# First loads padded by the host, decays and output weights first on the SyncE queue, gate columns copied by VectorE

## The chip, the cores and the metric

The kernel runs on one core of a Trainium2 chip. The time is device microseconds for one execution of the whole program, and the median of several executions is quoted. The profiled execution is one further run, with a time of its own.

## The reference

Three stages in float32 follow each other. The first is a linear recurrence over 768 steps for 4 batches and 8 heads of size 48:

```python
cur = einsum('bhd,bhe->bhde', u[None] * kt, vt)
y[:, :, t] = einsum('bhd,bhde->bhe', rt, state + cur)
state = wt[:, :, :, None] * state + einsum('bhd,bhe->bhde', kt, vt)
```

The second takes the 3072 resulting rows of 384 numbers through a dense layer: `a = x @ w1`, `b = x @ w2`, `h = a * b @ w3`, `h @ w_out`. The third is a mixture of 8 experts with a noisy top-2 choice: `logits = x @ w_gate`, `noise_scale = log1p(exp(x @ w_noise))`, and for each token the two largest of `logits + noise_scale * noise` choose the experts, each `relu(x @ w1[e]) @ w2[e]`, added with softmax weights.

## The kernel before, in words

**Attention.** Two heads make a pair (HP = 4 pairs a batch); head h of a pair lies on partitions 64h to 64h+47, since HB = 64 and D = 48. For each pair the kernel loads the decays w, the keys k and the receptance r turned (48 rows of 768 time steps a head) into `wt`, `kt`, `rt`, each with two buffers. The rows 48 to 63 of both heads are never loaded; a clearing at the start writes 1.0 over the whole of all six buffers (VectorE the three first buffers at L618, GpSimd the three second ones at L611), and the first load of a buffer waits for its clearing (`turned_clear`, L145). The time axis is cut into NC = 6 chunks of 128. VectorE scans the decays (`dve_decays`, L257), takes their inverse (L268), forms `kdiv` (L275) and `rdec` (L281), and from the row tiles `kn` and `rn` the diagonal `diag` (L292, L298, L307). ScalarE spreads `diag` over `att` (L320), TensorE makes the scores in two halves (L189), VectorE masks them into `att` (L328). TensorE turns the keys (L198), ScalarE copies them to `kend_t` (L248), TensorE multiplies them with the values (`pe_state`, L210), and states and outputs follow (L234, L240).

**The start-up.** While the first batch's attention runs, the weights are prepared. w3 and w_out are multiplied ahead of time, together with 2E = 16 gate columns. `front` does: six turns of w_out blocks (`wo_turn`, L655, copied by ScalarE to `woT`, L575), the product of w_out with the gate matrices (`wo_gates`, L664, copied at L583), and the turning back of that (`gates_turn`, L671), which ScalarE copies into the columns DM to WA of `wo` (L586, raising `wo_ready`). `build` then has 32 quarters `w3_mm` (L679): eight blocks `w3T` of w3, two buffers, each block in four quarters of two matmuls. The block q + 2 is loaded after the last quarter of block q (L545), in SyncE's program order, so behind other loads.

**Order.** All engines run lists written out at build time. `threaded` puts the main steps between attention slots; every engine walks the same list in the same order and does its own share of each step. At the start the list is: derive 0 (scan), two turns, derive 1, a turn, derive 2, a turn, derive 3 and 4, two turns, derive 5, diag 0, `wo_gates`, diag 1 and 2, four spreads, `gates_turn`; then the scores' first half, the turned keys, the first w3 quarter, the scores' second half, the state product, and so on. So ScalarE's copy of the gate columns comes behind the four spreads of three ACTIVATE each, and the second half of the scores comes behind the first w3 quarter on TensorE.

**Queues.** SyncE issues nearly all transfers, in one order: wt, kt, rt of pair 0, w3T block 0, kn, rn, u, the values, w3T block 1, the same of pair 1 with the first w1 blocks. ScalarE issues w_out (two halves of 768 KB) and the gate matrices on its own queue at the very start.

After the first batch the group loop begins (L793 and L810: the dense layer, with the attention of the next batch between), and then the experts (L1222, L1238).

Of the kernel before, what the change touches and what calls it, by code (L numbers as in the profile page):

```python
# [5 lines left out]
B, H, S, D = 4, 8, 768, 48  # L6
DM = H * D
# [50 lines left out]
def program(nc, w_turned, k_turned, r_turned, k_rows, r_rows, v_rows, u, w1, w2, w3_turned, w_out, gate_rows, noise_rows, ew1, ew2_rows, out):  # L58
# [10 lines left out]
    with top:  # L69
# [49 lines left out]

        xr_loaded = [asem("xr_loaded0")]  # L120
        consts_ready, ident_ready, small_loaded, pad_zero = (sem(x) for x in ("consts_ready", "ident_ready", "small_loaded", "pad_zero"))
        turned_clear = [sem(f"turned_clear{i}") for i in range(2)]
        ones_ready, cleared = sem("ones_ready"), sem("cleared")
        pool_waited = sem("pool_waited")
        loaded = [[sem(f"{x}_loaded{i}") for i in range(2)] for x in "wkr"]
# [15 lines left out]

        def sp_input_load(sp, b, q, n):
            g, i = HP * b + q, q % 2
            if g < 2:
                sp.wait_ge(turned_clear[g], n + 1)  # L145
            else:
                sp.wait_ge((decay_ready, kdiv_ready, rdec_ready)[n], g - 1)
            for h in range(2):
                sp.dma_start((wt, kt, rt)[n][i][h * HB:h * HB + D, :],
                             (w_turned, k_turned, r_turned)[n][bass.ds(b, 1), 2 * q + h, :, :].rearrange("o d t -> (o d) t")  # L150
                             ).then_inc(loaded[n][i], 16)

        def sp_rows_load(sp, b, q):
# [338 lines left out]
        with ExitStack() as ph:  # L492
# [24 lines left out]
            def first_sp(sp):  # L517
                def load_w3(n):
                    need(sp, wa_full, n - 1)
                    sp.dma_start(w3T[n % 2][:, :, :].rearrange("p m j -> p (m j)"), w3_turned[n, :, :]).then_inc(w3_loaded[n % 2], 16)  # L520

                def load_w12(n):
                    m, kk = divmod(n, KD)
                    if n >= 2:
                        sp.wait_ge(w12l_ready, n - 1)
                    sp.dma_start(wraw[n % 2][:, :], (w1, w2)[m][kk * P:(kk + 1) * P, :]).then_inc(wraw_loaded[n % 2], 16)

                for n in range(3):
                    sp_input_load(sp, 0, 0, n)
                load_w3(0)  # L530
                sp_rows_load(sp, 0, 0)
                sp.dma_start(u_all[:, :, :, :].rearrange("p q h d -> p (q h d)"),
                             bass.AP(u.tensor, u.offset, [[0, P], [1, H * D]])).then_inc(small_loaded, 16)
                sp_values_load(sp, 0, 0)
                load_w3(1)
                for n in range(3):
                    sp_input_load(sp, 0, 1, n)
                sp_rows_load(sp, 0, 1)
                load_w12(0)
                sp_values_load(sp, 0, 1)  # L540
                load_w12(1)
                for step, q, n in order:
                    if step == "w3_mm" and n == 3:
                        if q + 2 < KF:
                            load_w3(q + 2)  # L545
                        if 1 <= q < 2 * KD - 1:
                            load_w12(q + 1)
                    elif step == "derive" or step == "diag":
                        sp_attention(sp, 0, step, q, n)
                    elif step == "out":  # L550
                        sp_attention(sp, 0, step, q, n)
                        if (q, n) == (1, 0):
                            sp.wait_ge(pads_ready, 1)
                            sp.dma_start(slot_entry.rearrange("(p a n) o -> p a (n o)", p=P, a=PADS),
                                         pads[:, :, :].rearrange("p n o -> p (n o)").rearrange("p (a x) -> p a x", a=1)
                                         .broadcast_to([P, PADS, PADS * WORDS])).then_inc(pads_stored, 16)
                            sp.wait_ge(zeros_ready, 1)
                            sp.dma_start(x2[N:N + 1, :].rearrange("o (h d) -> o h d", h=2),
                                         zeros[0:1, :].rearrange("p (h d) -> p h d", h=1).broadcast_to([1, 2, DM // 2])).then_inc(row_cleared, 16)
                        if (q, n) == (HP - 1, 1):  # L560
                            for parity in range(2):
                                sp.wait_ge(y_stored[parity], 32 * HP)
                            sp.dma_start(turned_in, xa[:, 0:TG].rearrange("(k p) t -> p k t", p=P)).then_inc(xr_loaded[0], 16)

            def first_act(act):
                for part in range(2):
                    nc.scalar.dma_start(wo[:, 4 * part:4 * part + 4, 0:DM],
                                        w_out[part * F1 // 2:(part + 1) * F1 // 2, :].rearrange("(m p) d -> p m d", p=P)
                                        ).then_inc(wo_loaded[part], 16)
                nc.scalar.dma_start(gates[:, :, 0:2 * E], gate_rows[:, :, :]).then_inc(gates_loaded, 16)  # L570

                def evacuate(n):

                    act.wait_ge(wb_full, n + 1)
                    nc.scalar.copy(woT[:, n % KD, (n // KD) * 512:(n // KD + 1) * 512], bank[n % 2][:, :]).then_inc(wb_free, 1)  # L575

                for step, q, n in order:
                    act_attention(act, 0, step, q, n)
                    if step == "wo_turn":
                        evacuate(q)  # L580
                    elif step == "wo_gates":
                        act.wait_ge(gates_full, 1)
                        nc.scalar.copy(gates_side[:, :], fx[:, 0:2 * P]).then_inc(gates_out, 1)  # L583
                    elif step == "gates_turn":
                        act.wait_ge(gates_full, 2)
                        nc.scalar.copy(wo[:, :, DM:WA].rearrange("p (j t) e -> p t j e", t=2),  # L586
                                       fx[:, 2 * P:4 * P].rearrange("p (t j e) -> p t j e", t=2, j=4)[:, :, :, 0:2 * E]
                                       ).then_inc(wo_ready, 1)
                    elif step == "w3_mm" and n == 1 and 1 <= q <= 2 * KD:

                        m, kk = divmod(q - 1, KD)
                        act.wait_ge(wraw_loaded[(q - 1) % 2], 16 * ((q - 1) // 2 + 1))
                        nc.scalar.copy(w12h[:, m, kk, :], wraw[(q - 1) % 2][:, :]).then_inc(w12h_ready, 1)
                    elif step == "w3_mm" and n == 3:
                        act.wait_ge(wa_full, q + 1)
                        nc.scalar.copy(wah[:, q, :], sums[q % 2][:, 0:WA]).then_inc(wah_ready, 1)
                for part in range(2):
                    act_turn(act, 0, 0, part)

            def first_pool(pool):  # L600
# [6 lines left out]
                for i in range(2):  # L607
                    nc.gpsimd.memset(state[i][:, :, D:HB], 0.0).then_inc(pad_zero, 1)
                nc.gpsimd.memset(gates[:, :, 2 * E:4 * E], 0.0).then_inc(gates_clear, 1)
                for x in (wt, kt, rt):  # L610
                    nc.gpsimd.memset(x[1][:, :], 1.0).then_inc(turned_clear[1], 1)  # L611
                nc.gpsimd.memset(zeros[:, :], 0.0).then_inc(zeros_ready, 1)
                nc.gpsimd.memset(pads[:, :, 1:WORDS], 0)
                nc.gpsimd.memset(pads[:, :, 0:1], N).then_inc(pads_ready, 1)

            def first_dve(dve):
                for x in (wt, kt, rt):
                    nc.vector.memset(x[0][:, :], 1.0).then_inc(turned_clear[0], 1)  # L618
                nc.vector.memset(taken[:, :, :], 0.0)
                for i in range(2):  # L620
                    nc.vector.memset(decay[i][:, :, 0:1], 1.0).then_inc(cleared, 1)
# [6 lines left out]
                dve.wait_ge(consts_ready, 1)  # L628
                for step, q, n in order:
                    dve_attention(dve, 0, step, q, n)  # L630
                    if step == "w3_mm" and n == 2 and 1 <= q <= 2 * KD:

                        m, kk = divmod(q - 1, KD)
                        dve.wait_ge(w12h_ready, q)
                        nc.vector.tensor_tensor(w12l[:, m, kk, :], wraw[(q - 1) % 2][:, :], w12h[:, m, kk, :].bitcast(f32),
                                                ALU.subtract).then_inc(w12l_ready, 1)
                    elif step == "w3_mm" and n == 0 and q:
                        low(q - 1)
# [1046 lines left out]
def laid_out(np, inputs):  # L1685

    a = {name: np.asarray(x) for name, x in inputs.items()}

    def rows(x, pad):
        x = x.reshape(B, HP, 2, NC, P, D).transpose(0, 1, 4, 3, 2, 5)  # L1690
        return np.pad(x, [(0, 0)] * 5 + [(0, pad)])

    return {
        "w": a["w"].transpose(0, 1, 3, 2), "k": a["k"].transpose(0, 1, 3, 2), "r": a["r"].transpose(0, 1, 3, 2),
        "k_rows": rows(a["k"], 0), "r_rows": rows(a["r"], 0), "v_rows": rows(a["v"], HB - D), "u": a["u"],
        "moe_w1": a["moe_w1"], "moe_w2": a["moe_w2"],
        "moe_w3": a["moe_w3"].reshape(KF, P, KF, P).transpose(0, 3, 2, 1).reshape(KF, P, F1),
# [23 lines left out]
```

## Time and profile before

| what | us |
|---|---|
| median of 3 runs | 993.55 (992.33 to 994.73) |
| profiled execution | 987.84 |
| its span, first to last instruction | 986.1 |
| TensorE busy (matmul) | 950.7, 96% |
| weight loads | 895.8, 91% |
| VectorE busy | 677.8, 69% |
| ScalarE busy | 528.9, 54% |
| GpSimd busy | 226.4, 23% |

The span is the time between the first and the last instruction on the core; the profiled execution's time is 1.74 us longer than its span. Busy time of TensorE is modelled, so 96% does not say that it works at its peak. The page's row of slices shows TensorE at 9 tenths in all slices but the first two and the last, and the granted clock at 9 or 8 tenths in the first two and the last. In all 179.02 MB are moved at 182 GB/s on average.

### The profile page before, as it was taken

How to read it: one execution, taken by the hardware profiler on the slowest of the kernel's cores; microseconds unless marked ns; L12 is line 12 of the kernel's file. 1: busy time of each engine (PE TensorE's matmuls, PEld its weight loads, DVE VectorE, ACT ScalarE, POOL GpSimd, SP SyncE). 2: the span in 40 equal slices, each digit the busy share in tenths (PEclk: the TensorE clock that was granted, in tenths of full speed). 3: DMA queues.
4: the chain of work that ended last, by engine and by line, in shares of the span. 5: the costliest groups of instructions: out<-in, count | busy, mean ns of one | idle time of the engine just before them, and what ended most of it. 6: DMA issues, size and time to landing. Idle time of an engine off the chain costs nothing.

```text
span 986.1 us, 18066 instructions
## 1 busy us (share of the span) xinstructions
PE 950.7 (96%) x6825; PEld 895.8 (91%) x6825; DVE 677.8 (69%) x1135; ACT 528.9 (54%) x987; POOL 226.4 (23%) x212
## 2 busy tenths in 40 slices
PE   4989999999999999999999999999999999999995
PEld 2655899989998999999999999999999999999995
DVE  5799877969696967256776776746866568566570
ACT  3455444555554645325654666746756557565560
POOL 1000000010202020221454223333233332324321
PEclk9899999999999999999999999999999999999998
DMA  9887434353536120316458897877968779787751
GB/s 275 238 273 217 146 95 127 106 177 83 153 87 169 61 75 20 100 52 215 161 153 236 222 304 207 242 259 199 312 202 242 264 202 296 211 245 260 203 157 17
DMA packets 93451, 179.02 MB, mean 182 GB/s; under 512 B 18914, under 2 KB 50404, under 8 KB 93364
## 3 DMA queue, kind: packets, MB, share of 16 engines
q1 hardware_dynamic: 78932, 155.61, 50.5%
q0 software_dynamic: 12976, 20.66, 10.1%
q10 hardware_dynamic: 1456, 1.60, 0.6%
q8 instruction: 54, 0.88, 0.4%
q14 instruction: 33, 0.27, 0.1%
HBM read 152.22 MB, written 26.97 MB: 182 GB/s over the span
## 4 chain that ended last, share of the span: by engine, by line
PE 86%; DVE 5%; DMA 3%; ACT 3%; issue 1%; SPq 0%; POOL 0%; DVEq 0%; ACTq 0%; POOLq 0%
PE bank L1222 20%; PE pp L1238 20%; PE bank L793 13%; PE fx L793 6%; PE bank L810 6%; PE yu L1281 3%; PE fx L810 3%; PE pp L189 2%; PE tr L1203 2%; PE yu L1263 1%; PE fx L1263 1%; DMA tokens<-attention_out 1%; DVE kdiv L268 1%; PE yu L210 1%; PE bank L679 1%
## 5 line engine op out<-in xcount | busy, mean ns | idle before, releaser
L1132 POOL DMA_INDIRECT result<-x2s,who x55 | 93.5, 1700 | 283.4 <-ACT x2s L1355 259.1
L1342 DVE SCALAR_TENSOR_TENSOR abl<-bank,abh 128x512 fp32r<-128x512 f32 x96 | 66.2, 690 | 109.9 <-ACT abh L1337 109.9
L983 POOL DMA_INDIRECT slot_entry<-entry,slot_i x48 | 50.3, 1047 | 339.4 <-DVE token_f L972 327.2
L1222 PE MATMUL bank<-xh,set_up_h 128*128 128x256 f32 x384 | 109.2, 284 | 0.0
L1222 PE MATMUL bank<-xh,set_up_l 128*128 128x256 f32 x384 | 108.6, 283 | 0.0
L1222 PE MATMUL bank<-xl,set_up_h 128*128 128x256 f32 x384 | 108.6, 283 | 0.0
L1337 ACT ACTIVATE abh<-bank 128x512 fp32r<-128x512 f32 x96 | 57.5, 599 | 81.6 <-PE bank L1222 81.4
L793 PE MATMUL bank<-xh,w12h 128*128 128x384 f32 x264 | 89.5, 339 | 3.1 <-DVE xl L489 3.1
L793 PE MATMUL bank<-xh,w12l 128*128 128x384 f32 x264 | 88.4, 335 | 0.0
L793 PE MATMUL bank<-xl,w12h 128*128 128x384 f32 x264 | 88.2, 334 | 0.0
L1238 PE MATMUL pp<-set_down_h,abh 128*128 128x384 f32 x256 | 87.7, 342 | 0.0
L1238 PE MATMUL pp<-set_down_h,abl 128*128 128x384 f32 x256 | 85.7, 335 | 0.0
L1238 PE MATMUL pp<-set_down_l,abh 128*128 128x384 f32 x256 | 85.6, 334 | 0.0
L1119 POOL DMA_INDIRECT tokens<-ffn_out,who x55 | 76.4, 1389 | 33.4 <-issue 22.0
L268 DVE RECIPROCAL kdiv<-decay 128x256 f32<-128x256 f32 x48 | 82.2, 1733 | 0.3
L1222 PEld LDWEIGHTS bank<-xh,set_up_h 128*128 128x128 f32 x384 | 73.5, 191 | 0.5 <-DVE abl L1342 0.2
L1222 PEld LDWEIGHTS bank<-xl,set_up_h 128*128 128x128 f32 x384 | 73.5, 192 | 0.3
L1222 PEld LDWEIGHTS bank<-xh,set_up_l 128*128 128x128 f32 x384 | 73.5, 191 | 0.0
L1355 ACT ACTIVATE x2s<-pp,who 128x384 f32<-128x384 f32 x48 | 28.0, 582 | 84.3 <-PE pp L1238 79.3
L320 ACT ACTIVATE att<-ident,diag 128x128 f32<-128x128 f32 x192 | 59.5, 389 | 19.2 <-DVE diag L307 19.2
L1310 DVE TENSOR_TENSOR set_up_l<-up_raw,set_up_h 128x1024 fp32r<-128x1024 f32 x48 | 57.6, 1223 | 9.5 <-ACT set_up_h L1305 9.5
L1310 DVE TENSOR_TENSOR set_down_l<-down_raw,set_down_h 128x768 fp32r<-128x768 f32 x64 | 57.9, 953 | 4.0 <-ACT set_down_h L1305 3.7
(260 smaller groups left out, 2646.9 us busy)
## 6 DMA issues: line engine op xcount, KB each, us to landing
up_raw<-in_moe_w SPq DMA_DIRECT2D x93, 512.0 KB, 4.7
down_raw<-in_moe_w SPq DMA_DIRECT2D x124, 384.0 KB, 5.1
vs<-in_v_rows SPq DMA_DIRECT2D x16, 384.0 KB, 3.6
wt<-in_w SPq DMA_DIRECT2D x32, 144.0 KB, 2.9
kt<-in_k SPq DMA_DIRECT2D x32, 144.0 KB, 3.0
rt<-in_r SPq DMA_DIRECT2D x32, 144.0 KB, 3.2
kn<-in_k_rows SPq DMA_DIRECT2D x16, 288.0 KB, 3.3
rn<-in_r_rows SPq DMA_DIRECT2D x16, 288.0 KB, 4.3
```

The lines of the kernel that those rows point to most:

```text
L268: nc.vector.reciprocal(kdiv[q % 2][:, :].rearrange("p (c x) -> p c x", c=NC)[:, two, :], decay[q % 2][:, two, 1:C + 1]).then_inc(inverse_r ...
L320: last = nc.scalar.activation(att[:, j, h, c, :], ident[:, :], ACT.Copy, scale=diag[:, 3 * j + c, h:h + 1])
L793: last = nc.tensor.matmul(half_bank[n % 3][:, 0:TG], wp[:, m, kk, f * P:(f + 1) * P], xp[:, kk, :], start=(p == 0), stop=(p == 3 * KD - 1))
L810: last = nc.tensor.matmul(sum_at[s][:, 0:WA], xp[:, f, s * P:(s + 1) * P], wp[:, f, :], start=(f == 0 and n == 0), stop=(f == KF - 1 and n ...
L983: nc.gpsimd.indirect_dma_start(slot_entry, bass.IndirectOffsetOnAxis(slot_i[:, s, n:n + 1], 0), entry[:, s, n, :], None).then_inc(scattere ...
L1119: nc.gpsimd.indirect_dma_start(xg[v % 2][:, s, :], None, stored, bass.IndirectOffsetOnAxis(who[v % 4][:, s, 0:1], 0)).then_inc(gathered[v ...
L1132: nc.gpsimd.indirect_dma_start(out, bass.IndirectOffsetOnAxis(who[v % 4][:, s, 0:1], 0), yo[v % 2][:, s, 0:DM], None, bounds_check=N - 1, ...
L1222: last = nc.tensor.matmul(bank[m % 2][:, f * T2:(f + 1) * T2], wp[:, kk, c:c + P], xp[:, kk, :], start=(n == 0), stop=(n == 3 * KD - 1))
L1238: last = nc.tensor.matmul(pp[:, s, 0:DM], xp[:, f, s * P:(s + 1) * P], wp[:, f, :], start=(f == 0 and n == 0), stop=(f == KF - 1 and n == 2))
L1310: nc.vector.tensor_tensor(low, src, high.bitcast(f32), ALU.subtract).then_inc(w_low, 1)
L1337: nc.scalar.activation(hh[:, 2 * m:2 * m + 2, :].rearrange("p a t -> p (a t)"), bank[m % 2][:, :], ACT.Relu).then_inc(hh_ready, 1)
L1342: nc.vector.scalar_tensor_tensor(hl[:, 2 * m:2 * m + 2, :].rearrange("p a t -> p (a t)"), bank[m % 2][:, :], 0.0, hh[:, 2 * m:2 * m + 2, : ...
```

## The change

Four edits are made. The host lays out w, k and r with 64 rows a head, rows 48 to 63 filled with 1 for w and 0 for k and r. The first load of each buffer (g < 2) brings all 64 rows; later loads bring 48, as before. The six clearings and the semaphores for them are gone, so the first loads wait for nothing. The two loads of w_out move from ScalarE's queue to SyncE's, right behind the decays of pair 0; keys and receptance come after them. The copy of the gate columns from PSUM into `wo` moves from ScalarE to VectorE, at the same step of the list.

```diff
--- before.py
+++ after.py
@@ -119,7 +119,6 @@
 
         xr_loaded = [asem("xr_loaded0")]
         consts_ready, ident_ready, small_loaded, pad_zero = (sem(x) for x in ("consts_ready", "ident_ready", "small_loaded", "pad_zero"))
-        turned_clear = [sem(f"turned_clear{i}") for i in range(2)]
         ones_ready, cleared = sem("ones_ready"), sem("cleared")
         pool_waited = sem("pool_waited")
         loaded = [[sem(f"{x}_loaded{i}") for i in range(2)] for x in "wkr"]
@@ -141,13 +140,11 @@
 
         def sp_input_load(sp, b, q, n):
             g, i = HP * b + q, q % 2
-            if g < 2:
-                sp.wait_ge(turned_clear[g], n + 1)
-            else:
-                sp.wait_ge((decay_ready, kdiv_ready, rdec_ready)[n], g - 1)
+            rows = HB if g < 2 else D
+            need(sp, (decay_ready, kdiv_ready, rdec_ready)[n], g - 1)
             for h in range(2):
-                sp.dma_start((wt, kt, rt)[n][i][h * HB:h * HB + D, :],
-                             (w_turned, k_turned, r_turned)[n][bass.ds(b, 1), 2 * q + h, :, :].rearrange("o d t -> (o d) t")
+                sp.dma_start((wt, kt, rt)[n][i][h * HB:h * HB + rows, :],
+                             (w_turned, k_turned, r_turned)[n][bass.ds(b, 1), 2 * q + h, 0:rows, :].rearrange("o d t -> (o d) t")
                              ).then_inc(loaded[n][i], 16)
 
         def sp_rows_load(sp, b, q):
@@ -525,7 +522,12 @@
                         sp.wait_ge(w12l_ready, n - 1)
                     sp.dma_start(wraw[n % 2][:, :], (w1, w2)[m][kk * P:(kk + 1) * P, :]).then_inc(wraw_loaded[n % 2], 16)
 
-                for n in range(3):
+                sp_input_load(sp, 0, 0, 0)
+                for part in range(2):
+                    sp.dma_start(wo[:, 4 * part:4 * part + 4, 0:DM],
+                                 w_out[part * F1 // 2:(part + 1) * F1 // 2, :].rearrange("(m p) d -> p m d", p=P)
+                                 ).then_inc(wo_loaded[part], 16)
+                for n in (1, 2):
                     sp_input_load(sp, 0, 0, n)
                 load_w3(0)
                 sp_rows_load(sp, 0, 0)
@@ -563,10 +565,6 @@
                             sp.dma_start(turned_in, xa[:, 0:TG].rearrange("(k p) t -> p k t", p=P)).then_inc(xr_loaded[0], 16)
 
             def first_act(act):
-                for part in range(2):
-                    nc.scalar.dma_start(wo[:, 4 * part:4 * part + 4, 0:DM],
-                                        w_out[part * F1 // 2:(part + 1) * F1 // 2, :].rearrange("(m p) d -> p m d", p=P)
-                                        ).then_inc(wo_loaded[part], 16)
                 nc.scalar.dma_start(gates[:, :, 0:2 * E], gate_rows[:, :, :]).then_inc(gates_loaded, 16)
 
                 def evacuate(n):
@@ -581,11 +579,6 @@
                     elif step == "wo_gates":
                         act.wait_ge(gates_full, 1)
                         nc.scalar.copy(gates_side[:, :], fx[:, 0:2 * P]).then_inc(gates_out, 1)
-                    elif step == "gates_turn":
-                        act.wait_ge(gates_full, 2)
-                        nc.scalar.copy(wo[:, :, DM:WA].rearrange("p (j t) e -> p t j e", t=2),
-                                       fx[:, 2 * P:4 * P].rearrange("p (t j e) -> p t j e", t=2, j=4)[:, :, :, 0:2 * E]
-                                       ).then_inc(wo_ready, 1)
                     elif step == "w3_mm" and n == 1 and 1 <= q <= 2 * KD:
 
                         m, kk = divmod(q - 1, KD)
@@ -607,15 +600,11 @@
                 for i in range(2):
                     nc.gpsimd.memset(state[i][:, :, D:HB], 0.0).then_inc(pad_zero, 1)
                 nc.gpsimd.memset(gates[:, :, 2 * E:4 * E], 0.0).then_inc(gates_clear, 1)
-                for x in (wt, kt, rt):
-                    nc.gpsimd.memset(x[1][:, :], 1.0).then_inc(turned_clear[1], 1)
                 nc.gpsimd.memset(zeros[:, :], 0.0).then_inc(zeros_ready, 1)
                 nc.gpsimd.memset(pads[:, :, 1:WORDS], 0)
                 nc.gpsimd.memset(pads[:, :, 0:1], N).then_inc(pads_ready, 1)
 
             def first_dve(dve):
-                for x in (wt, kt, rt):
-                    nc.vector.memset(x[0][:, :], 1.0).then_inc(turned_clear[0], 1)
                 nc.vector.memset(taken[:, :, :], 0.0)
                 for i in range(2):
                     nc.vector.memset(decay[i][:, :, 0:1], 1.0).then_inc(cleared, 1)
@@ -628,7 +617,12 @@
                 dve.wait_ge(consts_ready, 1)
                 for step, q, n in order:
                     dve_attention(dve, 0, step, q, n)
-                    if step == "w3_mm" and n == 2 and 1 <= q <= 2 * KD:
+                    if step == "gates_turn":
+                        dve.wait_ge(gates_full, 2)
+                        nc.vector.tensor_copy(wo[:, :, DM:WA].rearrange("p (j t) e -> p t j e", t=2),
+                                              fx[:, 2 * P:4 * P].rearrange("p (t j e) -> p t j e", t=2, j=4)[:, :, :, 0:2 * E]
+                                              ).then_inc(wo_ready, 1)
+                    elif step == "w3_mm" and n == 2 and 1 <= q <= 2 * KD:
 
                         m, kk = divmod(q - 1, KD)
                         dve.wait_ge(w12h_ready, q)
@@ -1686,12 +1680,15 @@
 
     a = {name: np.asarray(x) for name, x in inputs.items()}
 
+    def turned(x, fill):
+        return np.pad(x.transpose(0, 1, 3, 2), [(0, 0), (0, 0), (0, HB - D), (0, 0)], constant_values=fill)
+
     def rows(x, pad):
         x = x.reshape(B, HP, 2, NC, P, D).transpose(0, 1, 4, 3, 2, 5)
         return np.pad(x, [(0, 0)] * 5 + [(0, pad)])
 
     return {
-        "w": a["w"].transpose(0, 1, 3, 2), "k": a["k"].transpose(0, 1, 3, 2), "r": a["r"].transpose(0, 1, 3, 2),
+        "w": turned(a["w"], 1), "k": turned(a["k"], 0), "r": turned(a["r"], 0),
         "k_rows": rows(a["k"], 0), "r_rows": rows(a["r"], 0), "v_rows": rows(a["v"], HB - D), "u": a["u"],
         "moe_w1": a["moe_w1"], "moe_w2": a["moe_w2"],
         "moe_w3": a["moe_w3"].reshape(KF, P, KF, P).transpose(0, 3, 2, 1).reshape(KF, P, F1),
```

## Rows read from the trace of the kernel before

**Rows 1.** Windows (`A:B`, length, busy and count per engine, PEclk, DMA share, GB/s).
```profile
0.00:20.30 20.30, 10.04 (x65) 6.89 (x66) 12.27 (x19) 5.18 (x8) 3.76 (x16) 1.00 0.93 266
...
3.00:5.00 2.00, 0.00 (x0) 0.00 (x0) 0.42 (x4) 0.83 (x1) 1.44 (x5) 1.00 1.03 388
...
8.00:12.00 4.00, 1.62 (x8) 1.23 (x7) 1.98 (x6) 0.83 (x2) 0.00 (x0) 1.00 1.11 202
...
18.00:22.00 4.00, 2.04 (x18) 1.46 (x17) 3.14 (x5) 0.76 (x3) 0.00 (x0) 0.79 1.03 214
...
20.30:33.90 13.60, 9.51 (x46) 5.71 (x44) 5.27 (x13) 6.26 (x20) 0.00 (x0) 0.50 0.93 273
...
33.00:45.50 12.50, 12.50 (x84) 7.58 (x83) 12.00 (x15) 6.50 (x17) 0.00 (x0) 0.96 0.67 197
...
101.00:900.00 799.00, 794.60 (x5760) 771.35 (x5761) 559.48 (x977) 442.50 (x812) 195.38 (x144) 1.00 0.60 177
```
**Rows 2.** Chain of waits, 0 to 130 us: start, duration, what.
```profile
10.02 2.01 DVE decay L257 x6
...
12.05 4.99 DVE kdiv L268 x3
...
21.24 3.61 ACT att L320 x12
...
25.15 3.00 PE fx L679 x4
```
**Rows 3.** Timeline, 0 to 40 us: start, duration, engine, line, operation, idle before.
```profile
0.83 1.00 ACTq L567 DMA_DIRECT2D wo<-in_moe_w_out  x2
...
1.77 0.87 SPq L149 DMA_DIRECT2D wt<-in_w  x2
...
4.84 0.42 SPq L520 DMA_DIRECT2D w3T<-in_moe_w  x1
...
5.68 2.88 PE L655 MATMUL bank<-ident,wo 128*128 128x128 f32 x12 [5.68 <-DMA wo<-in_moe_w_out]
...
10.93 2.90 PE L655 MATMUL bank<-ident,wo 128*128 128x128 f32 x12 [2.38 <-DMA wo<-in_moe_w_out]
...
17.65 0.44 PE L671 MATMUL fx<-ident,gates_side 128*128 128x128 f32 x2 [0.50 <-ACT gates_side L583]
...
18.88 0.75 DVE L292 TENSOR_TENSOR ruk<-kn,rn 128x576 f32<-128x576 f32 x1
...
19.11 0.94 PE L189 MATMUL pp<-rdec,kdiv 48*128 48x128 f32 x12 [1.02 <-DVE rdec L281]
...
24.76 0.24 ACT L586 COPY wo<-fx 128x128 f32<-128x128 f32 x1
...
28.08 1.65 PE L189 MATMUL pp<-rdec,kdiv 48*128 48x128 f32 x12
...
29.66 1.31 PE L210 MATMUL yu<-vs,kend_t 128*64 128x48 f32 x20
...
39.89 0.56 DVE L625 TENSOR_TENSOR wal<-fx,wah 128x400 fp32r<-128x400 f32 x1
```
**Rows 4.** Timeline, 40 to 100 us, third w3T block and the products around.
```profile
40.22 0.44 SPq L520 DMA_DIRECT2D w3T<-in_moe_w  x1
...
45.92 1.51 PE L679 MATMUL fx<-wo,w3T 128*128 128x400 f32 x4
...
47.36 0.94 PE L189 MATMUL pp<-rdec,kdiv 48*128 48x128 f32 x12
...
48.41 1.02 DVE L328 COPY_PREDICATED att<-causal,pp 128x768 f32<-128x768 int32 x1 [0.77 <-PE pp L189]
```
**Rows 5.** Landing: w3T issued in 4.8:5.2, in 40:41, wt in 34:36.
```profile
DMA to landing us min/median/max: 9.3/9.3/9.3
...
DMA to landing us min/median/max: 5.3/5.3/5.3
...
DMA to landing us min/median/max: 2.6/2.8/2.9
```

## The prediction

> **What bounds the kernel now.** I read first the windows, to see where the engine that sets the end has room. From 101 to 900 us TensorE is busy for 794.60 of 799 us at full clock: nothing in the change touches that stretch, so the change can only move the moment at which it begins. Before it, TensorE is busy for 10.04 of the first 20.3 us and 9.51 of the next 13.6 [rows 1]. Whatever that start-up (the first four head pairs, the product of w3 and w_out) loses or gains is handed to the end one for one, because all later work hangs on it in order.
>
> So the chain of waits over the start-up came next. VectorE gets its first real work, the scans, at 10.02, when wt has landed, then makes 4.99 us of reciprocals; later ScalarE's 3.61 us of spreading are on it, then TensorE's first four w3 products at 25.15 [rows 2]. The timeline explains the two late starts. SyncE issues wt only at 1.77, behind a clearing by VectorE, while ScalarE has put w_out on its own queue at 0.83. And the copy of the gate columns (24.76, 0.24 us) stands on ScalarE behind the twelve spreads, although their transposes were done at 18.09; the first w3 product waits for it [rows 3]. The scores of the second half (28.08) wait behind that product in TensorE's order, and VectorE's second mask waits for them.
>
> The third reading is the DMA share. It is 0.93 up to 33.9 us, but 0.67 between 33 and 45.5, so 12.5 x 0.33 = 4.1 us of the transfer engines are unused there [rows 1]. The third w3T block is issued at 40.22 and lands 5.3 us later, at 45.5; the product that needs it starts at 45.92 [rows 4, 5]. There is no slack: if everything before it comes earlier, this block must too.
>
> **Part 1: no clearing, wt first.** Clearing by VectorE goes (three of about 0.7 us), but it ran while VectorE waited for wt: worth nothing itself. Its end released SyncE; SyncE can then issue at about 0.83, as ScalarE does, 0.9 us earlier. A pair of wt loads on an unloaded queue lands 2.6 and 2.9 us after its issues, which are 0.4 apart [rows 5]: 0.83 + 0.4 + 2.9 = 4.2, with 64 instead of 48 rows at most a third more of it, 5.2. I take 4.5 for the first scan, 5.5 earlier than 10.02. Scans (2.03) and reciprocals (4.99) then end at 11.6, keys and queries, each 0.95 with the issue gaps of before, at 13.6.
>
> **Part 2: who gets the queue.** w_out (1.57 MB) now lies between wt and kt, and twelve first loads grow by 48 KB each, 0.59 MB. By bytes, at the 214 GB/s at which the 48-row loads run from 18 to 22 us, the growth costs 2.8 us of the transfer engines; if a 64-row load takes no longer than a 48-row one, nothing. Below nothing: from 8 to 12 us, with both queues filled, only 202 GB/s moved [rows 1]. One after the other, w_out at 388 takes 4.1, six loads at 214 take 4.1, w3T (0.52 MB) 1.3: 9.5 us, against 11.5 from 2.6 until w3T landed at 14.1. So the extra e lies between -2.0 and +2.8; I take its middle, +0.4, since no row shows a 64-row load. (That landing is the first w3T's issue at 4.84 and its 9.3 us [rows 3, 5].)
>
> The Trainium skill bears on both ends. Its page SBUF — State Buffer, "Door 1: The DMA port swizzle", says that a partition 32 higher is on the same port, so that a 64-partition load is limited like a 32-partition one. The half rate of the 48-row loads beside w_out's agrees [rows 1]; by that rule the +2.8 is near 0, e is -2.0 to 0, and the sum would give about 6.2 us of gain instead of the 4.8 below. Against the change stands DMA: Bandwidth & Descriptors, "Issuing engines are not separate DMA queues": moving a transfer to another issuing engine saves only issue time. By it the -2.0 is not to be had, e is 0 to 2.8, and the gain 3.8.
>
> The keys are not late: at the middle they land before 11.6. The row tiles kn and rn, right behind the first w3T, are the next to be late. It landed at 14.1, and their 0.59 MB at 388 GB/s make 15.6; with half of the growth ahead of it (1.4) or the saving (-2.0) that is 13.6 to 17.0, I take 15.2. VectorE, ready at 13.6, waits 1.6 us. Products and sum took from 18.88 to 21.24, 2.4 us [rows 2, 3]: done at 17.6, 3.6 earlier than before.
>
> **Part 3: the gate columns.** w_out's first half was worked on from 5.68; with wt ahead of it (0.39 MB, 1.8 us, less the sharing of before) I take 6.7. The three turns of the first half take 3.5 (2.88 of matmuls and a copy out), so the second begins at 10.2, not 10.93, and from there to the transposes' end is 7.1 (10.93 to 18.09): 17.3. The copy by VectorE isn't in the trace; ScalarE's took 0.24, VectorE's subtraction of 400 columns from the same bank 0.56 (at 39.89), so 0.2 to 0.6, I take 0.3: ready at 17.9. Queued behind the copy on VectorE is the first mask, which waits for ScalarE's spreading until 19.5 anyway, so it is hidden; that cover is gone if w_out lands over 1.6 us later than I say. ScalarE's spreading goes 17.6 to 21.3, and the turned keys' copy (0.69) to 22.0.
>
> TensorE: scores 17.3, transposes until 19.3 (1.95 as from 19.11 to 21.06 [rows 3]), then the first w3 products, whose gate columns are there: not at 25.15 but at 19.3. At half clock they take 3.0, the second scores 1.6 and the state products 1.3, so 25.2 against 30.97: 5.8 earlier. At full clock (1.51 to 2.0, 0.94 [rows 4], and the 1.31 scaled as the scores, 0.8) it is 23.0, 8.0 earlier; the mask and the copy, due by 22.0, are no obstacle.
>
> **The cap.** Up to there 5.8 to 8.0 us are won, but the third w3T block can't come that much earlier. The transfers ahead of it are the same work; with all 4.1 us of unused time filled, and e = 0.4 more of work, it lands 3.7 earlier. As it was used 0.4 after its landing, TensorE's product moves from 45.92 to 41.9, 4.0 earlier. VectorE had 0.77 us to spare before the mask that follows [rows 4], so its own chain keeps 4.0 + 0.8 = 4.8. From then on VectorE is the bound (from 33 to 45.5 us it already worked 12.00 of 12.50, [rows 1]), transfers and issues move with it at the same distances, so nothing behind is late next.
>
> The sum: 4.8 us off. The profiled execution took 987.84 for a span of 986.1; it would have a span of 981.3. The median of the runs, 993.55, lies 5.7 above that execution; taken off it, the forecast is 988.7. With e at its ends the gain is 4.8 - 2.4 = 2.4 and 4.8 + 2.4 = 7.2: 986.3 to 991.2.
>
> **Rivals.**
> Bytes rule (18%): 64-row loads cost their bytes in full and the single queue saves nothing. e = 2.8, w3T moves only 1.6, VectorE's chain 2.4, 991.2; with the small stores in the way perhaps less. For it: no row shows a larger load of this kind run any faster. Against: at 214 GB/s, beside 388, something other than bytes limits them [rows 1].
>
> The cap doesn't bind (15%): ports take 64 rows for the price of 48 and the queue saves its 2 us. Then 7.2 is left, or the 8.0 of the front at full clock: 985.6 to 986.3. For it: 202 against 388 GB/s. Against: little is unused otherwise.
>
> Slower, by the clock (7%): TensorE has nothing to do until 6.7, and may be granted the lower level, 1.2 GHz, from there rather than from 20.3. Before, it fell there after 10.04 busy us in 20.3 and rose at 33.9 after unbroken work from 25.15 on [rows 1, 2]. Twelve scores take 1.65 at that level and 0.94 at the higher [rows 3, 4], a factor of 1.75. Of the 10.04 busy us up to 20.3, 8.9 come before the scores; they would cost 6.6 more, so 23.9 instead of 17.3, scores and transposes 3.4, and 5.9 for the rest: 33.2 against 30.97, 2.2 us later, 995.8. It decides once the lower level costs more than the 5.8 won at the front. Against it: the same idle start before left the clock high, and TensorE's work is now less broken.
>
> The gain is absorbed before 101 us by another order of transfers (5%): within 1 us of 993.
>
> The forecast itself has 55%, its own range 986.3 to 991.2.
>
> A difference of 0.2% is 2 us, about what a measurement tells here from none. Faster: 0.53 of the forecast's 0.55, half of the bytes rule's, all of the third: 0.78. Same: 0.15, slower 0.07. The runs of before spread by 1.2 either way, so the range goes from 985.3 to 992.6; outside are the slower case and the edges.
>
> **What would show it.** First scan at 4 to 5 us; products of rows starting with a wait on kn or rn at 13.5 to 17; the first w3 product at about 19, released by transposes or by VectorE's copy; state products ending 23 to 25; a new wait of TensorE on w3T near 40 us with the DMA share near 1 from 33 to 42; the stretch from 101 us on as long as before. It is wrong if kt or rt land after 13 (w_out ahead of them was too dear), if the DMA share between 33 and 42 stays low while w3T is late, or if the granted clock is at its lower level before 17 us.

## The result: slower by 0.42%

The changed kernel takes 997.39 us (median of 20 runs, 992.97 to 1003.16) against 993.41 for the kernel before in the same jobs (20 runs, 990.76 to 999.35): ratio 1.0042, 95% interval 1.0028 to 1.0056. The forecast was 988.7, with a range of 985.3 to 992.6. The profiled span is 995.0 us against 986.1.

The front of the kernel came early, if less than forecast (the state products by 3.7 us). TensorE's waits over the first 110 us (who waited for whom: total, times, longest) show where it was lost:

```profile
PE bank L649 <- DMA wo<-in_moe_w_out: 10.2, 2, 9.4
PE fx L673 <- DMA w3T<-in_moe_w: 7.1, 1, 7.1
```

The second row is new; before, all waits for w3T together were 1.5 us. The chain of waits (start, duration, what) puts it on the path:

```profile
36.47 12.59 DMA w3T<-in_moe_w
49.11 3.03 PE fx L673 x4
```

That is the third w3T block, issued at 36.47 instead of 40.22 [rows 4] and landed at 49.1 instead of 45.5. The timeline of the changed kernel, against [rows 2 to 4]:

```profile
0.82 1.22 SPq L146 DMA_DIRECT2D wt<-in_w  x2
...
4.46 2.37 SPq L146 DMA_DIRECT2D rt<-in_r  x2
...
5.47 2.00 DVE L254 TENSOR_TENSOR_SCAN decay<-wt 128x128 f32<-128x128 f32 x6 [4.46 <-DMA wt<-in_w]
...
9.42 2.88 PE L649 MATMUL bank<-ident,wo 128*128 128x128 f32 x12 [9.42 <-DMA wo<-in_moe_w_out]
...
14.72 0.96 DVE L272 TENSOR_TENSOR kdiv<-kt,kdiv 128x768 f32<-128x768 f32 x1 [2.23 <-DMA kt<-in_k]
...
19.11 0.76 DVE L289 TENSOR_TENSOR ruk<-kn,rn 128x576 f32<-128x576 f32 x1 [1.69 <-DMA rn<-in_r_rows]
...
21.36 0.28 DVE L622 COPY wo<-fx 128x128 f32<-128x128 f32 x1
...
23.31 2.36 PE L673 MATMUL fx<-wo,w3T 128*128 128x400 f32 x4
...
26.46 0.79 PE L207 MATMUL yu<-vs,kend_t 128*64 128x48 f32 x20
```

The state products end at 27.3 instead of 30.97. TensorE's 120th to 160th matmuls begin 5.2 us earlier than the same ones before; from the third block's product on, and nearly unchanged up to 400 us, they begin 4.8 us later. So 10 us were lost at one place: 3.2 us because the product starts at 49.11 instead of 45.92, another 1.5 because its four matmuls take 3.03 instead of 1.51, and the 5.2 already won. The windows (columns as in [rows 1]) show both causes:

```profile
33.00:40.00 7.00, 6.32 (x19) 3.23 (x17) 6.86 (x8) 4.21 (x12) 0.00 (x0) 1.00 1.04 229
...
45.50:51.00 5.50, 1.89 (x3) 1.17 (x4) 0.00 (x0) 0.00 (x0) 0.00 (x0) 0.50 1.03 265
```

From 33 to 40 us the transfer engines are busy without a break and move only 229 GB/s; the reader should set the share, 1.04, beside the rate: full, yet little over half of the 388 seen before from 3 to 5 us [rows 1]. And in the long wait TensorE's granted clock has gone to 0.50, its 1.2 GHz level, at which the product then runs.

The profiled spans differ by 8.9 us, the medians by 4.0. Setting each matmul beside the same one of before shows 4.7 to 5.0 of it before 410 us; 3.8 more come between 440 and 545 us. The two kernels are the same there, and the profile of e1, whose median is that of before, is also late there, by 5.0: the profiled execution of before (987.84) was a quick one in that stretch.

### The profile page after: what moved, and what is told of

Its sections match the earlier page's. It is cut to its first block, busy times and chain, and to the rows that moved or that the text cites. A ratio compares the mean times of both kernels' runs of the same rounds, so it can differ in the third digit from the quotient of the medians.

```text
span 995.0 us, 18060 instructions
## 1 busy us (share of the span) xinstructions
PE 951.6 (96%) x6825; PEld 895.5 (90%) x6825; DVE 676.4 (68%) x1133; ACT 528.2 (53%) x986; POOL 218.8 (22%) x209
## 4 chain that ended last, share of the span: by engine, by line
PE 86%; DVE 4%; DMA 3%; issue 2%; ACT 2%; SPq 1%; another core or an unknown queue 0%; POOL 0%; DVEq 0%; ACTq 0%; POOLq 0%
PE pp L1232 20%; PE bank L1216 19%; PE bank L787 13%; PE bank L804 7%; PE fx L787 6%; PE fx L804 4%; PE yu L1275 3%; PE pp L186 3%; DMA w3T<-in_moe_w 2%; PE tr L1197 2%; PE yu L1257 1%; PE fx L1257 1%; DMA wo<-in_moe_w_out 1%; PE yu L207 1%; PE yu L237 1%
## 5 line engine op out<-in xcount | busy, mean ns | idle before, releaser
L1113 POOL DMA_INDIRECT tokens<-ffn_out,who x55 | 72.0, 1310 | 31.4 <-issue 22.9
L1304 DVE TENSOR_TENSOR w12l<-up_raw,w12h 128x1024 fp32r<-128x1024 f32 x45 | 54.9, 1223 | 8.5 <-ACT w12h L1299 6.3
```

The lines of the kernel that those rows point to most:

```text
L1113: nc.gpsimd.indirect_dma_start(xg[v % 2][:, s, :], None, stored, bass.IndirectOffsetOnAxis(who[v % 4][:, s, 0:1], 0)).then_inc(gathered[v ...
L1304: nc.vector.tensor_tensor(low, src, high.bitcast(f32), ALU.subtract).then_inc(w_low, 1)
```

## Experiments

Edits are against the kernel named; w3T 3 is the landing of the third w3T block in the profile, in us (45.5 before). Each ratio is to the kernel before in the same job; between jobs the median of before itself lay between 988.89 and 993.41, so runs of different jobs are compared by their ratios alone.

| run | rows | w_out on | gate copy | w3T 3 | ratio, interval |
|---|---|---|---|---|---|
| before | 48 | ScalarE | ScalarE | 45.5 | 1 |
| changed | 64 | SyncE | VectorE | 49.1, 47.7 (e13) | 1.0042 (1.0028 to 1.0056) |
| e1 | 64 | ScalarE | ScalarE | 44.3 | 0.9998 (0.9982 to 1.0014) |
| e2 | 48 | SyncE | ScalarE | 42.7, 43.1 (e14) | 0.9985 (0.9961 to 1.0008) |
| e3 | 48 | ScalarE | VectorE | 41.6 | 0.9968 (0.9953 to 0.9983) |
| e4 | 48 | SyncE | VectorE | 45.8, 43.1 (e15) | 1.0014 (0.9997 to 1.0032) |
| e7 | 64 | ScalarE | VectorE | 45.3 | 0.9998 (0.9979 to 1.0017) |
| e8 | 64 | SyncE | ScalarE | 46.3 | 1.0036 (1.0016 to 1.0057) |
| e5 | one load of 128, first loads | SyncE | VectorE | 39.4 | 0.9948 (0.9932 to 0.9964) |
| e6 | one load of 128, all loads | SyncE | VectorE | 36.2 | 0.9925 (0.9906 to 0.9944) |
| e9 | as e5, cut in two by time | SyncE | VectorE | 41.0 | 0.9997 (0.9982 to 1.0012) |
| e10 | 64, one pause | SyncE | VectorE | 49.9 | 1.0072 (1.0053 to 1.0091) |
| e11 | e6, w_out by halves | SyncE | VectorE | 39.3 | 0.9963 (0.9949 to 0.9977) |
| e12 | e6, kn, rn, u ahead of w3T | SyncE | VectorE | 35.7 | 0.9914 (0.9895 to 0.9933) |
| e16 | 64, w_out ahead of wt | SyncE | VectorE | 45.1 | 0.9983 (0.9961 to 1.0004) |

A landing is that of one execution. For e7 and e16 the profiled one took 7.3 us longer than the median of its kernel's runs, so these two landings say less than their ratios.

**e1, the rows alone** (against before; the clearings and their waits go too; the slice of the source grows in the same way).

```diff
-                sp.dma_start((wt, kt, rt)[n][i][h * HB:h * HB + D, :],
+                sp.dma_start((wt, kt, rt)[n][i][h * HB:h * HB + rows, :],
...
```

> Only the 64-row first loads, no clearing; w_out on ScalarE's queue and the gate copy on ScalarE as before. Row theory (the 64-row loads take far more transfer time than their bytes and disturb the loads behind them): the third w3T block, landed at 45.5 us before and at 49.1 after the change, lands at 48 or later, ratio to before 1.003 to 1.005. Queue theory (w_out in the single queue, ahead of kt, is what costs): the block lands at 45 to 47, ratio 0.999 to 1.001.

**e2, the queue order alone.**

```diff
-                for n in range(3):
+                sp_input_load(sp, 0, 0, 0)
...
+                for n in (1, 2):
                     sp_input_load(sp, 0, 0, n)
```

> Only the order: wt, then w_out, then kt and rt, all on SyncE's queue; 48 rows and clearings as before, gate copy on ScalarE. Row theory: no loss, the third w3T block lands at 42 to 45.5, ratio 0.996 to 1.000. Queue theory: the block lands at 47 or later, ratio 1.002 to 1.005.

**e3, the gate copy alone** (the copy at `gates_turn` moved from `first_act` to `first_dve`).

> Only the gate copy on VectorE. Both theories: the first w3 product starts at about 21.5 us instead of 25.15, and the third w3T block can move by at most the unused transfer time; ratio 0.996 to 0.999. If the start-up is capped by transfers altogether: within 0.001 of 1.

**e4, the change without its rows** (48 rows, clearings kept).

> The whole change but the rows: 48 rows, clearings kept, w_out on SyncE's queue after wt, gate copy on VectorE. Row theory: the third w3T block lands at 41 to 44 us, ratio to before 0.995 to 0.998. Queue theory: it lands at 47 or later as in the changed kernel, ratio 1.002 to 1.005.

Taken singly, no edit makes the kernel slower: 0.9998, 0.9985 and 0.9968. Added up they should give 0.995; together they give 1.0042. Neither theory foresaw that. The gate copy is the one clear gain, and it behaves as predicted. Its first w3 product and its third block's issue in the timeline and the landing view:

```profile
21.63 1.88 PE L679 MATMUL fx<-wo,w3T 128*128 128x400 f32 x4
```
```profile
DMA to landing us min/median/max: 5.4/5.4/5.4
```

It is issued at 36.2 and lands at 41.6: the transfer time left unused before is filled, and the block comes as early as the cap said (41.4). Now the transfers have next to nothing to spare, and there each of the other two edits costs: from e3 to e7 (rows) 3.7 us of landing, from e3 to e4 (queue) 4.2, to the changed kernel 7.5.

The landing of this block is not the whole of the time. In e2 the matmuls around 48 us begin 3.1 us earlier than before, at 101 us they begin 0.3 later; in e5 5.3 us earlier shrink to 1.7. Both have a stretch at a lower clock behind a 2.5 us wait for `kdiv` (granted 0.67 from 60 to 66 us in e5, 1.00 before), and then a wait of 1.7 us for VectorE's next `kdiv` that the kernel before does not have. So part of what an early block wins is given back before the group loop.

**e7 and e8, the change without the queue order, and without the gate copy.**

> The changed kernel with w_out back on ScalarE's queue and kt, rt right behind wt; 64 rows and VectorE's gate copy kept. Step theory: the rows alone cost little as long as w_out comes first on a queue of its own; gain of the gate copy less the rows', ratio 0.996 to 0.999. Order theory: the same, 0.996 to 0.998. If the rows and the gate copy spoil each other: over 1.000.

> The changed kernel with the gate copy back on ScalarE: 64 rows, w_out on SyncE's queue. Both theories: the earlier need of the third w3T block isn't what costs, its late landing is, so this is as slow as the changed kernel, 1.002 to 1.006. If the gate copy's earlier demands cause the loss: 0.998 to 1.001.

e7 missed the 0.996 to 0.999 of both theories by a little: the rows, harmless in e1, take back the gate copy's whole gain, and the block lands 3.7 us later than in e3. e8 is slow as both theories said, 1.0036. It asks for the block no earlier than before (40.2), but its transfers are late from the front on, the first w3T block at 17.7 instead of 14.1. Yet some transfer time is still unused around its third block (compare 0.67 before, [rows 1]):

```profile
33.00:45.50 12.50, 11.39 (x84) 7.05 (x82) 12.32 (x16) 6.39 (x17) 0.00 (x0) 1.00 0.84 253
```

So the rows and the queue order lose together even without the gate copy's early demand; an overrun of the unused time alone does not explain that.

**e5 and e6, one load over 128 partitions** (against the changed kernel; in e6 for every pair, with the waits at 16 a load).

```diff
-            for h in range(2):
-                sp.dma_start((wt, kt, rt)[n][i][h * HB:h * HB + rows, :],
-                             ...[bass.ds(b, 1), 2 * q + h, 0:rows, :].rearrange("o d t -> (o d) t")
+            sp.dma_start((wt, kt, rt)[n][i][:, :],
+                         ...[bass.ds(b, 1), 2 * q:2 * q + 2, :, :].rearrange("o h d t -> (o h d) t")
```

> The changed kernel, but the first two loads of wt, kt and rt each bring both heads' 64 rows in one transfer over all 128 partitions instead of two over 64 (same bytes). Step theory (a load over one half of the partitions runs at about 214 GB/s and puts the 16 transfer engines out of step, so that the loads behind it run at 230 to 260 instead of 390): kt lands before 12 us, the third w3T block at 39 to 43, ratio to before 0.993 to 0.997. Order theory (w_out ahead of kt in one queue costs whatever the loads look like): the block lands at 46 or later, ratio 1.001 to 1.004.

> As the former, and the later loads of wt, kt and rt too are one transfer over 128 partitions (a third more bytes each, 64 rows instead of 48, half the issues). Step theory: the third w3T block lands at 38 to 41 us, the sixth no longer keeps TensorE waiting, ratio 0.991 to 0.996. Order theory: as the changed kernel or worse, 1.002 to 1.005.

Both came out as the step theory said, e6's block even earlier (36.2) than its 38 to 41. e5 moves exactly the bytes of the changed kernel in the first loads and is 0.9% faster than it, by the two ratios. In all the core has moved 12.44 MB when e5's third block lands at 39.4, and 12.94 when the changed kernel's does at 49.1: what differs is the rate far more than the bytes. The windows of e6, the same stretches as for the changed kernel and [rows 1]:

```profile
4.00:6.00 2.00, 0.00 (x0) 0.00 (x0) 1.39 (x5) 0.00 (x0) 0.00 (x0) 1.00 1.06 384
...
18.00:33.00 15.00, 13.58 (x105) 8.43 (x104) 12.51 (x19) 8.49 (x24) 0.00 (x0) 1.00 1.02 375
```

and of the changed kernel:

```profile
18.00:33.00 15.00, 14.51 (x125) 9.42 (x118) 9.67 (x18) 7.43 (x22) 0.00 (x0) 1.00 1.04 285
```

At the same share, 375 GB/s instead of 285. (e5, whose later loads come by halves again, moves 300 in this stretch.) Until the third block has landed, a packet takes (mean ns in the traces, by size; 3072 are wt, kt and rt, 4096 are w1 and w3, 2304 kn and rn):

```
              3072   4096   2304
before         193    181    116
changed        190    227    143
e5             157    170    122
e6             131    167     99
```

The packets of w3, which cover all partitions, pay too: in the changed kernel 227 against 167. The Trainium skill's page SBUF — State Buffer, "Door 1: The DMA port swizzle", says that 64 partitions of one half reach only 8 of the 16 ports. The 3072 column agrees: 190 against 131 ns. That the cost spreads to the loads beside them is seen in the 4096 column.

**e9, the same loads cut by time.**

```diff
+                for h in range(2):
+                    sp.dma_start((wt, kt, rt)[n][i][:, h * S // 2:(h + 1) * S // 2], ...
```

> The changed kernel; the first loads of wt, kt, rt stay two transfers of 192 KB each, but cut by time (128 partitions x 384 steps) instead of by head (64 partitions x 768 steps). Step theory (which partitions a load covers is what counts): as with one load for both heads, the third w3T block lands before 43 us, ratio 0.993 to 0.998. Issue theory (half as many issues, or the SyncE queue's slower issuing, made that gain): as slow as the changed kernel, 1.001 to 1.006.

Half right. The transfers run at full rate:

```profile
10.00:20.00 10.00, 8.50 (x67) 5.26 (x65) 5.48 (x7) 5.60 (x14) 0.00 (x0) 1.00 1.04 388
```

and the block lands at 41.0, but the time is 0.9997, not 0.993 to 0.998. About half of what e5 wins over the changed kernel is taken back (w_out's first half is there at 8.8 us instead of 6.8). Twice the issues and half-length packets are what e9 has beside e5; which of the two costs it was not separated.

**e10, a pause.** After rt of pair 1: `sp.wait_ge(loaded[2][1], 32)`.

> The changed kernel with one pause: SyncE waits until rt of pair 1 has landed before it issues on, so the transfer queues run empty once at about 27 us. Step theory (engines that got out of step get back into it only when the queues run empty): the loads behind run near 390 GB/s again and the third w3T block lands no later than the 49.1 of the changed kernel though about 2 us were left unused, 45 to 49; ratio below 1.004. Bytes theory (the transfers are simply too many): the pause adds its 2 us, the block lands at 51, ratio 1.005 to 1.008.

The step theory's claim that an empty queue cures it fell: 1.0072, inside the bytes theory's range, the block at 49.9, and from 34 to 39 us, with the next half-partition loads, the rate was down to between 197 and 235 GB/s.

**e11, w_out by halves of the partitions** (against e6).

```diff
+                    for h in range(2):
+                        sp.dma_start(wo[h * HB:(h + 1) * HB, 4 * part:4 * part + 4, 0:DM], ...
```

> The kernel with one load over 128 partitions for all of wt, kt, rt (0.9925), but each half of w_out now comes as two transfers over 64 partitions: same bytes, two issues more. Step theory: the 1.57 MB take 7.4 us at 214 GB/s instead of 4.1, w_out's second half and kt land about 3 us later, loads behind are mixed; slower than 0.9925 by 0.003 or more. Issue or order theory: within 0.001 of it.

The direct measurement of the disputed cost. From 4 to 9 us, while only w_out comes:

```profile
4.00:9.00 5.00, 0.00 (x0) 0.02 (x1) 4.42 (x8) 0.00 (x0) 0.00 (x0) 1.00 1.06 221
...
14.00:18.00 4.00, 2.72 (x32) 1.49 (x34) 2.08 (x3) 1.50 (x4) 0.00 (x0) 1.00 1.06 402
```

221 GB/s against 384 for the same bytes in e6, and the time goes from 0.9925 to 0.9963. From 14 us on, when no half-partition load is under way, the rate is 402: in e11 the cost ends with these loads.

**e12, the rows ahead of w3T** (against e6: `sp_rows_load` and u are issued before `load_w3(0)`).

> The kernel with one load over 128 partitions for all of wt, kt, rt, and the first w3T block issued behind kn, rn and u instead of ahead of them: VectorE's 0.9 us of waiting for u at 15 us goes, the first w3 product (17.2) still finds its block. 0.9 us better than the 0.9925 if the start-up is still led by that chain, 0.991 to 0.992; no difference if the group loop's start is set by something else behind.

The best version: 981.03 us against 989.44 of before in its job (5 and 22 runs), 0.86% faster. VectorE's wait for u is gone, and the group loop's first product starts at 93.13 us instead of 101.50 before and 95.43 in e6. By the runs it is not told apart from e6: the intervals overlap.

**e13 to e16, what the queue order does.**

> The changed kernel itself, a second execution under the profiler. If the late third w3T block is how this order always runs: landed at 47 to 51 us, at least 12.8 MB moved by then. If the first profile was an unlucky execution: at 42 to 46.

> The kernel with only the queue order changed, a second execution under the profiler. The first had the first w3T block landed at 13.7 us and the third at 42.7. If the order alone puts the transfer engines out of step in some executions and not in others (its timed runs lie 13.7 us apart, those of before 6.0): now one with the first block at 15 to 17 and the third at 45 or later, or again like the first. If it is always in step: the same to 0.5 us.

> The changed kernel with 48 rows and clearings, a second execution under the profiler. The first had the first w3T block at 16.0 us and the third at 45.8, though its program up to 18 us differs from the queue-only kernel's in nothing that transfers. If that is a matter of the execution: the first block can be at 13.7 this time, the third then at 42 to 43. If it belongs to the kernel: 16.0 and 45.8 again.

> The changed kernel with w_out ahead of wt on SyncE's queue, so that the 64-row loads of pair 0 follow each other without a break. Between theory (w_out in the middle of half-partition loads is what puts the engines out of step): the third w3T block lands at 43 to 46, as with w_out on ScalarE's queue (45.3), the first scan starts 3 to 4 us later than with wt first; ratio 0.998 to 1.001. Single-queue theory (all on one queue, wherever w_out stands): 47 to 50, ratio 1.002 to 1.006.

The changed kernel is late in both executions (49.1, 47.7). The queue order with 48 rows isn't settled by one profile: e4 and e15 are the same kernel and land the block at 45.8 and 43.1, so 1.5 to 4.2 us over e3. That part differs from one execution to the next (the two also ran on different chips); e15's first w3T block, at 14.4, came near e2's 13.7. e2 and e14 repeat to 0.4 us. The changed kernel had moved 12.6 MB at e13's landing, under the 12.8 expected. e16 lands it at 45.1 and is 0.9983: with w_out ahead of all half-partition loads the single queue costs little, about as on ScalarE's queue (e7: 0.9998), so it is w_out's place that costs, not the shared queue. (The scans start at 10.24 in it, 4.8 us later than with wt first, and it is still the faster.) Whether the engines get out of step inside the queue no view shows, since packets aren't listed by engine; why w_out's place costs stays open.

## Why the prediction was wrong, step by step

**The bound and the place** were right: the start-up alone moved, and the third w3T block capped it.

**Part 1** was nearly right in time: wt was issued at 0.82, the first scan began at 5.47, forecast 4.5. But issuing 0.95 us earlier won nothing. With 48 rows and the clearing kept (e14) wt is issued at 1.77, and the scan starts as early:

```profile
5.36 2.00 DVE L257 TENSOR_TENSOR_SCAN decay<-wt 128x128 f32<-128x128 f32 x6 [1.94 <-DMA wt<-in_w]
```

The 64-row pair took the time back, in issuing (1.22 us for the two instead of 0.87) and on the way. And kt landed at 14.7 and rn at 19.1, where I had said before 11.6 and 15.2, outside the 13.6 to 17.0 for rn. One of the prediction's signs, "It is wrong if kt or rt land after 13", came true.

**Part 2 is the step that failed**: "the extra e lies between -2.0 and +2.8; I take its middle, +0.4". The cap without e was 41.4, and e3 measured 41.6. The changed kernel landed the block at 49.1 and 47.7: e was 7.7 and 6.3. The rows cost about 3.3 and 4.6 of it (49.1 - 45.8, 47.7 - 43.1, differences of single executions; e7 less e3 gives 3.7), which looks more than their bytes' 2.8. The other bound, that a 64-row load takes no longer than a 48-row one, had nothing for it: 64 rows at a time run at 221 GB/s (w_out in e11, in packets of half the length), 48 at 214 [rows 1]. At an equal rate a third more bytes take a third more time; the prediction had read an equal rate as an equal time. For the queue I had allowed a saving of 2.0 or nothing; it cost 4.2 and 1.5. With 48 rows and the copy where it was (e2, e14) the first w3T block landed at 13.7 instead of 14.1, a saving of 0.4. The 2.0 were worked out by charging each load its own rate alone, 388 for w_out and 214 for the halves, one cleanly after the other. In the changed kernel w_out starts behind wt's halves, and from 4 to 6 us, when nearly all packets are its own, 189 GB/s move at a share of only 0.69; its first half came at 9.4 instead of the 6.7 forecast.

```profile
4.00:6.00 2.00, 0.00 (x0) 0.00 (x0) 0.53 (x2) 0.00 (x0) 0.00 (x0) 1.00 0.69 189
```

The row on which the saving rested was misread: 202 GB/s from 8 to 12 us [rows 1], taken as the price of two filled queues. In that stretch ScalarE's queue, w_out's (q10), carries 0.03 of the 0.81 MB (queue: packets, MB, share):

```profile
q1 hardware_dynamic: 319, 0.78, 100.5%
q10 hardware_dynamic: 326, 0.03, 10.5%
```

w_out was all but through (7 of its 1024 packets start after 8 us), and what ran at 202 were the half-partition loads themselves with the w3T block behind them. Such loads alone run at 221 (e11), one queue without them at 384 (e6). So there was hardly anything for a single queue to save. (Two queues without such loads were not run.) The rule of the Trainium skill's page DMA: Bandwidth & Descriptors, "Issuing engines are not separate DMA queues", that only issue time is saved, spoke against the saving; e2's and e14's 0.4 us agree with it, and the changed kernel goes further against the saving than the rule does.

**Part 3** was right in kind: the copy took VectorE 0.28 (forecast 0.3) and alone gives 0.9968. In the changed kernel the first product came at 23.3 rather than 19.3, for w_out and rn were late; 3.7 us were won by the state products' end instead of 5.8 to 8.0. And "nothing behind is late next" was too hopeful: in e3, where the block came as the cap said, the matmuls around 48 us begin 4.3 us earlier, those at 155 us 2.7, and the runs give 3.2 us (0.9968), not the 4.8 of the sum.

**The rivals.** The bytes rule (18%) was right that 64 rows cost their bytes and that the queue saves nothing, but with all of e at 2.8 it still forecast a gain (991.2). The slower case (7%) was a fall of the clock at the front. It fell later, in the 7 us wait, as a consequence worth 1.5 us; that this case's 995.8 came nearest to the measured time is luck. No rival was an e beyond the bounds, and that was the mistake of the range: both ends of e came from pure rates and no row read for it held a w_out load among halves. Two slips change nothing: 1.2 on either side of 986.3 to 991.2 is 985.1 to 992.4, and the chances of faster add up to 0.77.

**The size by the end.** 4.8 us at the group loop are 0.48%, the measured 0.42%.

## What to carry to other kernels

Where several edits draw on one resource, price them together and not one by one: here each was harmless or better alone, and every pair gave less than its parts promised (e4, e7, e8). The traces point to two causes, the unused transfer time (4.1 us) that the gate copy alone already fills (e3), and w_out's place among the half-partition loads (e16); their shares were not separated. Load over all 128 partitions in one transfer if the layout allows it; padding the heads to 64 rows paid only once it was used for that (e5, e6, e12). And before a low rate is put down to two queues, look at what each of them carried in that stretch.

## What the runs showed of the hardware

w_out over 64 partitions at a time runs at 221 GB/s (e11), the same bytes over 128 at 384 (e6). While such loads are in the queues, packets of full-width loads are slower as well (227 against 167 ns for 4096 bytes). In a wait of 7.1 us TensorE's granted clock fell to 0.50 (1.2 GHz), and the next four matmuls took 3.03 us instead of 1.51. The two 64-row loads of wt took 1.22 us to issue, the two of 48 rows 0.87. A full busy share of the transfer engines (1.02 to 1.06) was seen at 221, 229, 285, 375 and 402 GB/s: it does not tell the rate.
